# Moving small groups of TensorE work inside an order written out by hand: retention, an MLP and a routed expert layer in one kernel

## The reference, cut to what matters

```python
# 1: retention, 4 x 8 heads of 64, 768 steps
state = gamma * state + outer(k[t], v[t]);  y[t] = scale * q[t] @ state
# 2: an MLP of width 2048
h = x @ w_in;  r = maximum(h, 0);  g = s * r * r + b;  x = g @ w_out
# 3: 8 experts, 384 tokens each, chosen greedily over all (token, expert) logits in falling order
logits = x @ w_gate
out[mask_e] = maximum(x[mask_e] @ w1[e], 0) @ w2[e]
```

## Time and profile before

| | us |
|---|---|
| median of 3 runs | 937.32 (937.30 to 937.77) |
| the profiled execution | 938.31 |
| its span in the trace | 936.5 |
| PE busy | 925.5 (99%) |
| VectorE, ScalarE, GpSimd busy | 514.7, 296.0, 234.6 |
| granted TensorE clock over the span | 0.999 |

### The profile page before, as it was taken

How to read it: one execution, slowest core, us unless ns; L and a number is a source line. 1 busy time by engine, 2 the same in 40 slices (tenths; PEclk the granted TensorE clock), 3 DMA queues, 4 the chain that set the end, 5 groups by cost and what they waited for, 6 DMA issues and landing times.

```text
span 936.5 us, 18563 instructions
## 1 busy us (share of the span) xinstructions
PE 925.5 (99%) x7461; PEld 748.1 (80%) x7461; DVE 514.7 (55%) x1218; ACT 296.0 (32%) x557; POOL 234.6 (25%) x216
## 2 busy tenths in 40 slices
PE   8999999999999999999999999999999999999997
PEld 6777777778777777777777777778898998999996
DVE  6776566565665465467676676761534434424420
ACT  3453444343443452010101010101434534534421
POOL 5222222222222000001110101001443643643611
PEclk9999999999999999999999999999999999999999
DMA  9986657666665468767676767284635635635500
GB/s 337 316 311 229 243 215 256 222 231 227 244 229 193 182 245 304 258 206 225 213 233 195 246 202 228 85 273 133 224 109 184 200 116 180 203 120 172 180 34 34
DMA packets 81317, 192.93 MB, mean 206 GB/s; under 512 B 8880, under 2 KB 17584, under 8 KB 81232
## 3 DMA queue, kind: packets, MB, share of 16 engines
q1 hardware_dynamic: 77200, 178.98, 56.8%
q0 software_dynamic: 3840, 12.59, 4.1%
q10 hardware_dynamic: 192, 0.19, 0.1%
HBM read 128.54 MB, written 63.18 MB: 205 GB/s over the span
## 4 chain that ended last, share of the span: by engine, by line
PE 95%; DMA 2%; DVE 2%; issue 1%; ACT 0%; POOLq 0%; SPq 0%; POOL 0%; DVEq 0%
PE bank L1180 28%; PE bank L1065 28%; PE bank L1221 14%; PE bank L1236 14%; PE bank L998 3%; PE bank L908 1%; PE bank L1200 1%; PE bank L932 1%; PE bank L896 1%; PE bank L867 1%; PE bank L1096 1%; DMA staging<-in_w_in 1%; PE bank L872 1%; PE bank L968 0%; DVE w_lo L1613 0%
## 5 line engine op out<-in xcount | busy, mean ns | idle before, releaser
L1065 PE MATMUL bank<-x,wi_hi 128*128 128x512 f32 x768 | 240.8, 395 | 0.0
L1065 PEld LDWEIGHTS bank<-x,wi_hi 128*128 128x128 f32 x768 | 141.7, 188 | 45.4 <-issue 10.9
L691 POOL TENSOR_TENSOR w_lo<-w_raw,w_hi 128x512 fp32r<-128x512 f32 x72 | 94.4, 1320 | 289.5 <-ACT w_hi L806 289.3
L1065 PE MATMUL bank<-x,wi_lo 128*128 128x512 f32 x384 | 149.6, 390 | 0.0
L1180 PE MATMUL bank<-wo_b,g_back 128*128 128x512 f32 x552 | 137.6, 399 | 0.0
L1307 DVE SCALAR_TENSOR_TENSOR u_sb<-u_sb,cst 128x512 f32<-128x512 f32 x96 | 78.8, 821 | 100.4 <-ACT u_sb L736 100.4
L806 ACT ACTIVATE w_hi<-w_raw 128x512 fp32r<-128x512 f32 x128 | 76.6, 636 | 163.6 <-DMA w_raw<-in_w 163.0
L736 ACT ACTIVATE u_sb<-bank 128x512 f32<-128x512 f32 x96 | 57.4, 598 | 185.4 <-PE bank L1065 185.4
L1180 PEld LDWEIGHTS bank<-wo_b,g_back 128*128 128x128 f32 x552 | 99.5, 189 | 18.5 <-issue 0.8
L1613 DVE TENSOR_TENSOR w_lo<-w_raw,w_hi 128x512 fp32r<-128x512 f32 x56 | 62.4, 1114 | 67.7 <-ACT w_hi L806 67.7
L1608 DVE SCALAR_TENSOR_TENSOR e_lo<-bank,e_hi 128x384 fp32r<-128x384 f32 x64 | 35.4, 553 | 95.3 <-ACT e_hi L844 95.3
(11 more groups left out here) (209 smaller groups left out, 1185.8 us busy)
## 6 DMA issues: line engine op xcount, KB each, us to landing
g_rows<-g_sb SPq DMA_DIRECT2D x96, 512.0 KB, 3.0
g_back<-g_rows SPq DMA_DIRECT2D x80, 512.0 KB, 3.9
w_raw<-in_w SPq DMA_DIRECT2D x128, 256.0 KB, 3.7
x_rows<-x SPq DMA_DIRECT2D x25, 256.0 KB, 5.0
g_back<-g_rows SPq DMA_DIRECT2D x16, 384.0 KB, 4.5
kT<-in_k_turned SPq DMA_DIRECT2D x22, 256.0 KB, 3.8
qT<-in_q_turned SPq DMA_DIRECT2D x22, 256.0 KB, 3.8
vin<-in_v SPq DMA_DIRECT2D x22, 256.0 KB, 4.1
```

Source lines behind the costliest of these rows:

```text
L691: pool.tensor_tensor(low, w_raw[:, (p * E_PIECES + n) % RAW, :], high.bitcast(F32), ALU.subtract).then_inc(w1_lo_done, 1)
L1065: last = pe.matmul(up[i % 2][:, :], w[:, t, fs], x[:, half, t, :], start=(t == 0 and n_ == 0), stop=(t == DT - 1 and n_ == 2))
```

## The change

Six edits of TensorE's order; the mathematics stays.

```diff
-FIRST_SCORE_AT = 1
+FIRST_SCORE_AT = 2
-FIRST_QUAD_AT = {4: 0, 11: 1, 14: 2}
+FIRST_QUAD_AT, LAST_QUADS_AT = {4: 0, 11: 1, 14: 2}, 8
-LATE_TURN_AT = {len(DOWN_UNITS) - 6: 0, len(DOWN_UNITS) - 4: 1}
+LATE_TURN_AT = {len(DOWN_UNITS) - 5: 0, len(DOWN_UNITS) - 3: 1}
-LIST_AT, RANK_AT, OWNED_AT = 34, 37, 41
+RANK_AT, OWNED_AT = 37, 41
-    if _r:
-        ROUTE[_at + LIST_AT] = ("list", _r - 1, 0)
-TURNS = {36 + 6 * j: j for j in range(CT)}
+TURNS_AT = 36
...
-                    if f in quads:
+                    if blk < N_BLK - 1 and f in quads:
                         quad(blk, quads[f])
+                    if blk == N_BLK - 1 and f == LAST_QUADS_AT:
+                        quad(blk, 0)
+                        quad(blk, 1)
...
                 pe.matmul(vote_ps, unit16[:, k_, :], full16[:, :], start=(k_ % HIGH == 0), stop=True,
                           skip_group_check=True).then_inc(vote_done, 1)
+                if r and k_ == PASSES - 1:
+                    list_tokens(r - 1)
...
                 if unit == END_QUAD:
+                    quad(N_BLK - 1, QUADS - 2)
                     quad(N_BLK - 1, QUADS - 1)
...
-                    if p + 1 < EXPERTS and u_ in TURNS:
-                        turn_tokens(p + 1, TURNS[u_])
+                    if p + 1 < EXPERTS and u_ == TURNS_AT:
+                        for j in range(CT):
+                            turn_tokens(p + 1, j)
```

## The result

The changed kernel took 942.12 us (median of 5 runs, 941.77 to 943.29) against 937.32 before (5 runs): ratio 1.0053, 95% interval 1.0041 to 1.0064, so 4.8 us slower. The forecast was 939.5 with a range to 941.5: the sign was right, the size was under half. The profiled execution took 943.29, its span is 941.5.

What follows compares the result with a forecast made beforehand. TensorE's work in order was taken to bound the kernel. Two new waits, 2.56 + 1.43, less 1.77 saved gave +2.2 us; on 937.32 that made 939.5, range 937.7 to 941.5.

Steps and rivals of the forecast that it cites:

- the first wait: Block 0, TensorE at w_og_parts(0): waits for mask(4), now behind square(2) on VectorE; group 3 2.56 us late.
- the second: Block 0, increment(5) on TensorE: waits for decay_k(5), late through add_second(4) and ageing; 1.43 us more.
- the clock falls in the first wait: Rival, block 0: TensorE drops to the lower clock level, adding 1.5 to 2.7 us, 941.5; chance 0.08.
- The argument against it: Program end: TensorE does nothing from 930 to 934, yet the granted clock is still 1.00.
- Quads: Last block: quads put together two by two share edges, 4.16 instead of 4.48 us; 0.32 saved.
- First turnings: One down unit later, turn_first(0) no longer waits for its gather; 0.65 us saved; turn_first(2) might become late.
- Turnings of the experts: Expert turnings joined: 14 edges go, each little more than 0.01 us; 0.2 us saved.
- Lists: Routing: six lists placed behind votes each lose a bf16 group's edge of 0.10 us; 0.60 us saved.
- The base: The earlier kernel's profiled execution, 938.31 us, taken as 1.0 above its median; the forecast started from 937.32.
- the transfers catch up: Rival, block 0: later TensorE gives keys more time, small waits (some 0.6 us) go; +1.6, 938.9; chance 0.12.

Runs made afterwards that it cites:

- the increment alone: The kernel before with only FIRST_SCORE_AT set to 2, moving the increment as in the changed kernel: 943.86 us, ratio 1.0066.
- the second wait removed: The changed kernel with add_second(4) on VectorE directly behind add_state(4): 941.11 us, ratio 1.0038 to the kernel before.
- VectorE's order mended: The changed kernel with add_state(3), mask(4), add_state(4) and add_second(4) earlier on VectorE, TensorE's order as changed: 936.45 us, ratio 0.9986 to the kernel before.
- the version without the parts' wait: The changed kernel without the wait for mask(4) ahead of w_og_parts(0): 937.33 us, ratio 0.9994 to the kernel before.
- the lists alone: The kernel before with only the lists moved behind the votes: 937.41 us, ratio 0.9999.
- the version with the increment put back: The changed kernel with the increment again behind group 1 (FIRST_SCORE_AT = 1), all else as changed: 936.15 us, ratio 0.9984 to the kernel before.
- the version with eight fillers: The changed kernel with eight bf16 matmuls, whose result nobody reads, in TensorE's wait before w_og_parts(0): 941.01 us, ratio 1.0035 to the kernel before.
- the one with twelve: The changed kernel with twelve bf16 matmuls, whose result nobody reads, in TensorE's wait before w_og_parts(0): 941.71 us, ratio 1.0042 to the kernel before.
- the changed kernel again: A repetition of the changed kernel with nothing altered: 942.25 us, ratio 1.0052 to the kernel before.
- four fillers: The changed kernel with four bf16 matmuls, whose result nobody reads, in TensorE's wait before w_og_parts(0): 941.25 us, ratio 1.0041 to the kernel before.

## Why the prediction was wrong

The sum's terms for the moved increment held: the first wait 2.51 (2.56 forecast), the second 1.43 (1.43), once the clock is taken out by filler. The step that failed is the rival "the clock falls in the first wait": it had a chance of 0.08 and was put at nothing in the sum. It happened in every profiled execution that has the wait of 3.2 us (the changed kernel twice, the increment alone, the second wait removed) and, by the mean clocks, in all runs of the changed kernel. It costs 1.6 to 2.9 us, which the rival's own bounds, 1.5 to 2.7, nearly held; it was the likeliest case and was priced as a remote one.

The argument against it took one stretch, the idle end of the program in the earlier trace rows, as proof that four idle microseconds are survived. The same view of the kernel before goes on, and one row further the clock is at half: it fell at 934.98, 5.1 us behind the last matmul.

```profile
934.00:935.00 1.00, 0.00 (x0) 0.00 (x0) 0.00 (x0) 0.00 (x0) 0.00 (x0) 0.99 0.00 0
935.00:936.50 1.50, 0.00 (x0) 0.00 (x0) 0.00 (x0) 0.00 (x0) 0.00 (x0) 0.50 0.00 0
```

So that trace showed already that idling lowers the clock here, and left open only how soon. The thirteen traces now show that this time is no constant: from the last matmul to the fall of the clock it is 5.1 us in the kernel before, 3.1 in the changed one and 1.95 in the version with VectorE's order mended. The rule of the Trainium skill (TensorE: Matmul & The Clock Gate, "The HAM clock gate"), that idling halves the clock, holds here: granted clock 0.50 after a break of 3.2 us. It should have outweighed the two rows.

Point by point:
- *Quads*: 0.35 saved, 0.32 forecast.
- *First turnings*: 0.73, 0.65 forecast; turn_first(2) did not wait. As said.
- *Turnings of the experts*: 0.02 over six experts, against 0.2 for seven. The forecast's own 14 edges of 0.01 make 0.14. The first matmul behind the turnings still starts late; there was no edge to share.
- *Lists*: 0.60 forecast. The edges are 0.08 to 0.10 in five rounds and 0.02 in one, and 0.3 of them is given back in the fourth round, where TensorE, earlier by what it saved, waits for VectorE. In the trace of the changed kernel without the moved increment the routing gains 0.14 in all. In that of the changed kernel it loses 0.37, but the increment alone, with its lists where they were, loses 0.59 there: most of this is chance of the execution, not the lists.
- *The base*: the profiled execution of before lost 0.69 at 66, where the increment came late, and 0.5 around 662. Beside it every other trace but that of the version without the parts' wait gains just these two amounts at these places, also the increment alone and the lists alone, which change nothing there. The first of them is a late transfer of keys, read on GpSimd: the scaling starts when they land, ends at 67.00, and the increment follows 0.10 later.

```profile
65.96 1.04 POOL L620 TENSOR_TENSOR kin<-kin,cst 128x512 f32<-128x512 f32 x1 [2.67 <-DMA kin<-in_k]
```

  With these two the changed kernel looked 1.2 better beside that execution than it is, and with the luck in the routing some 0.5 worse; the net is near the 1.0 by which that execution lay above the median. The rival "the transfers catch up" explained the first by a later TensorE; the version with the increment put back lacks it too, so it was chance.

The size without the clock is less sure than its two large terms. With the savings as traces show them (0.35, 0.73, 0.02, 0.14) it is 3.94 - 1.24 = 2.7, where the forecast had 2.2. By the times the version with eight fillers is 3.3 slower (2.1 to 4.5), the one with twelve 3.9 (2.6 to 5.2). The 2.7 lies within both intervals, the forecast's 2.2 in the first alone. That the forecast without the clock would have come close is likely, then, but not shown to better than a microsecond.

## What to carry to other kernels

When one constant moves work on two engines, write out the second engine's order as well: here the edit on TensorE was harmless, and the same number put a mask behind the very group it should overlap. Price a new wait on TensorE not only by its length but by what the clock does behind it: here a break of 3.2 us was enough in every execution looked at, one of 2.2 in two runs of four. When a row of an idle stretch speaks against a fall, read the rows behind it as well. Joining small groups saves only the edge that the trace shows: nothing to speak of behind the turnings (0.02 over six experts), and little where another engine is as late. And look in a second trace before you count on a small wait in the first; of this kernel's one profiled execution, 1.2 us were chance.

## What the runs showed of the hardware

The granted clock fell at different points around the same wait of 3.2 us. It was 2.5 us into the break (33.45, changed kernel, and 33.93, the increment alone), just as work resumed (33.89 against 33.83, the second wait removed), or 1.6 us after that (35.59 against 34.02, the changed kernel again). It stayed low 6.83 us in the first two and 3.41 in the others. At the start of the program it rose between 4.3 and 10.0 us into the span, TensorE's first matmul being at 1.08 in every trace; the late rise (four fillers) shifts the first large matmul by 1.1 us.

A few VectorE operations last much longer than others of their line, such as

```profile
521.02 1.27 DVE L1446 TENSOR_SCALAR folded<-top 128x24 int32<-128x24 int32 x1
```

which otherwise lasts 0.18. In the routing of each trace there are three to six that last over 0.35 us longer than the median of their line. Their cause was not tried.
